# Where three groups of VectorE sums stand in a fast-matrix-product feed-forward kernel

## The reference

```python
def _moe_ref(x, w_in, w_out):             # the second layer: 1.702 * h in the exponent
    h = x @ w_in                          # 2304x512 @ 512x2048
    g = h * (1.0 / (1.0 + np.exp(-h)))
    return (g @ w_out).astype(np.float32) # 2304x2048 @ 2048x512
...
x = np.ascontiguousarray(attn_out.transpose(0, 2, 1, 3)).reshape(B * S, H * D)
x = _moe_ref(x=x, **moe_kwargs)
return _moe2_ref(x=x, **moe2_kwargs)
```

## Time and profile before

| | before |
|---|---|
| median of 3 runs | 829.08 us (828.62, 829.08, 831.41) |
| the profiled execution, its own time | 831.32 us |
| its span, first to last instruction | 829.4 us |
| TensorE matmul busy | 806.5 us (97%) |
| VectorE busy | 653.4 us (79%) |
| ScalarE busy | 536.2 us (65%) |
| GpSimd busy | 191.8 us (23%) |
| TensorE's mean granted clock | 0.994 |
| DMA | 205.42 MB, mean 248 GB/s |

### The profile page before, as it was taken

How to read it: one execution, slowest core, us unless ns; L and a number is a source line. 1 busy time by engine, 2 the same in 40 slices (tenths; PEclk the granted TensorE clock), 3 DMA queues, 4 the chain that set the end, 5 groups by cost and what they waited for, 6 DMA issues and landing times.

```text
span 829.4 us, 15638 instructions
## 1 busy us (share of the span) xinstructions
PE 806.5 (97%) x5787; PEld 778.4 (94%) x5787; DVE 653.4 (79%) x945; ACT 536.2 (65%) x865; POOL 191.8 (23%) x191
## 2 busy tenths in 40 slices
PE   7988899999999999999999999999999999999998
PEld 4766679999999999999999999999999999999997
DVE  6889869989989867888767888899756677665465
ACT  5887775667735567745677555687465787365763
POOL 6678768612025511036300000000000000000000
PEclk8999999999999999999999999999999999999999
DMA  7878756877677897768887787877887777878773
GB/s 211 246 196 231 200 163 234 276 245 260 205 247 249 274 311 263 251 209 262 265 288 254 232 258 251 271 244 235 301 282 260 265 252 265 290 241 267 270 260 126
DMA packets 98315, 205.42 MB, mean 248 GB/s; under 512 B 8416, under 2 KB 56032, under 8 KB 98240
## 3 DMA queue, kind: packets, MB, share of 16 engines
q1 hardware_dynamic: 98240, 204.42, 75.5%
HBM read 160.87 MB, written 43.52 MB: 246 GB/s over the span
## 4 chain that ended last, share of the span: by engine, by line
PE 76%; DVE 8%; DMA 6%; issue 3%; POOL 3%; ACT 2%; SPq 0%; DVEq 0%; POOLq 0%; ACTq 0%
PE hid L322 39%; PE yp L345 35%; DMA vn<-in_v 5%; DVE gr L498 2%; POOL vpair L897 2%; DMA wr<-in_w_in 1%; DVE wh L294 1%; DVE xs L255 1%; PE pt L1090 1%; ACT xs L251 1%; ACT wh L285 0%; DVE x L1063 0%; ACT yt L938 0%; POOL pband L900 0%; ACT pavg L988 0%
## 5 line engine op out<-in xcount | busy, mean ns | idle before, releaser
L322 PE MATMUL hid<-xs,wh 128*128 128x384 f32 x2016 | 352.9, 335 | 3.2 <-DVE hw L478 2.1
L322 PEld LDWEIGHTS hid<-xs,wh 128*128 128x128 f32 x2016 | 349.0, 188 | 6.1 <-issue 4.8
L345 PE MATMUL yp<-gr,wh 128*128 128x384 f32 x2016 | 352.5, 335 | 1.8 <-DVE gr L498 1.8
L345 PEld LDWEIGHTS yp<-gr,wh 128*128 128x128 f32 x2016 | 351.0, 189 | 2.3 <-issue 2.3
L285 ACT ACTIVATE wh<-wr 128x1024 fp32r<-128x1024 f32 (+1 forms) x164 | 164.5, 1003 | 157.7 <-PE hid L322 118.0
L498 DVE TENSOR_TENSOR gr<-G,gr 128x768 fp32r<-128x768 f32 x144 | 138.6, 971 | 48.3 <-ACT gr L398 48.2
L398 ACT ACTIVATE gr<-G 128x768 fp32r<-128x768 f32 x144 | 121.8, 846 | 68.9 <-PE yp L345 67.6
L294 DVE TENSOR_TENSOR wh<-wr,wh 128x1024 fp32r<-128x1024 f32 x76 | 89.4, 1176 | 23.1 <-ACT wh L285 23.0
L365 ACT ACTIVATE G<-G 128x1152 f32<-128x1152 f32 x48 | 55.8, 1162 | 0.0
L488 DVE TENSOR_TENSOR G<-hv,hid 128x384 f32<-128x384 f32 x48 | 26.5, 552 | 27.0 <-PE hid L322 26.9
L473 DVE TENSOR_TENSOR hv<-p,hid 128x384 f32<-128x384 f32 x48 | 26.4, 549 | 26.9 <-PE hid L322 19.3
(11 more groups left out here) (94 smaller groups left out, 766.8 us busy)
## 6 DMA issues: line engine op xcount, KB each, us to landing
wh<-rests SPq DMA_DIRECT2D x72, 512.0 KB, 3.8
wr<-sums_out SPq DMA_DIRECT2D x48, 512.0 KB, 4.7
wr<-in_w_out SPq DMA_DIRECT2D x36, 512.0 KB, 5.2
rests<-wh SPq DMA_DIRECT2D x36, 512.0 KB, 3.3
wr<-sums_in SPq DMA_DIRECT2D x40, 384.0 KB, 4.0
wr<-in_w_in SPq DMA_DIRECT2D x40, 256.0 KB, 3.4
qk<-in_qkT SPq DMA_DIRECT2D x11, 576.0 KB, 6.3
G<-in_w_in SPq DMA_DIRECT2D x12, 512.0 KB, 7.2
```

Of the source, the lines that this page charges most:

```text
L322: last = eng.matmul(hid[:, at, 0:HALF], lhsT=wh[:, w % SLOTS, part, a % 4, cc * P:(cc + 1) * P], rhs=xs[:, rest, q, cc, :], start=start an ...
L345: last = eng.matmul(yp[:, at + m, 0:HALF], lhsT=wh[:, w % SLOTS, part, p % 4, m * P:(m + 1) * P], rhs=gr[:, p, rest, :], start=start and p ...
```

## The change

`results` moves on VectorE from the end of product 6's list to its head. On ScalarE the last `round_x` of the next block moves from behind a weight rounding to before it, in the same product. In blocks 0 and 3 three of the four slices of `sum_t2` move into the first phase (behind the G22 sum of pairs 2, 4 and 6), the fourth goes to product 1 of the second phase, and the four slices of `sum_t4` move from product 4 to products 2 and 3, where `sum_t2` was. No instruction is added or removed.

```diff
@@ scalar: second(n, i)
+                if i == 6:
+                    round_x(eng, n + 1, FILLS[i])
                 for a in range(4):
                     if i < 6:
                         round_gates(n, i + 1, a)
                     if a == 1:
                         round_weights(eng, w + SLOTS)
-                    if a == 2:
+                    if a == 2 and i < 6:
                         round_x(eng, n + 1, FILLS[i])
...
+        EARLY_T2 = (0, 3)
...
@@ vector: first(n, p)
                 eng.tensor_tensor(G[:, p, G22, :], hw[:], hid[:, 3, 0:HALF], ALU.add).then_inc(self.h_sum, 1)
+                if n in EARLY_T2 and p in (2, 4, 6):
+                    sum_t2(n, p // 2 - 1)
                 rest_weights(eng, w + SLOTS)
...
@@ vector: second(n, i)
+                if i == 6:
+                    results(n)
                 for a in range(4):
                     if i < 6:
                         rest_gates(n, i + 1, a)
                     if a == 1:
                         rest_weights(eng, w + SLOTS)
-                        if 2 <= i < 4:
+                        if n in EARLY_T2:
+                            if 2 <= i < 4:
+                                sum_t4(n, 2 * i - 4)
+                        elif 2 <= i < 4:
                             sum_t2(n, 2 * i - 4)
                         elif i == 4:
                             sum_t4(n, 0)
                     if a == 2:
                         prepare_x(eng, n + 1, i)
                     if a == 3:
-                        if 2 <= i < 4:
+                        if n in EARLY_T2:
+                            if i == 1:
+                                sum_t2(n, 3)
+                            elif 2 <= i < 4:
+                                sum_t4(n, 2 * i - 3)
+                        elif 2 <= i < 4:
                             sum_t2(n, 2 * i - 3)
                         elif i == 4:
                             for b in range(1, 4):
                                 sum_t4(n, b)
-                if i == 6:
-                    results(n)
                 rest_weights(eng, w + 1 + SLOTS)
```

## The result

The changed kernel takes **824.73 us** (median of 6 runs, 823.02 to 825.78); the kernel before, beside it, 828.8 us (6 runs, 827.47 to 831.41). The ratio is 0.9948, with a 95% interval of 0.9928 to 0.9968: faster by 0.5%. The forecast was 824.7 us, with a range of 822.9 to 827.8. The total came out as forecast, but the terms behind it didn't all.

The account below looks back on a forecast made before the run. TensorE's matmuls fill 97% of the span, so only its lost 7.83 us can be won. Terms of 3.5, 0.2, 0.8, 0.8, 0.3 and 0.8 sum to 6.4 us; between 824.9 and 824.4 it took 824.7 us, range 822.9 to 827.8.

Parts of the forecast that it names:

- The T2 and T4 sums in block 0: Block 0, second phase: TensorE's gap at product 6 goes and the slow clock with it; 3.5 us, bounds 1.8 to 3.6.
- Rival 1: Block 0, second phase: the gap is won but the clock falls anyway, 1.7 us not won; 826.4 us, chance 0.10.
- the forecast's two workings: Total: 824.9 us from the profiled execution less 6.4; 824.4 from the median less 4.7, if it lacked the slow clock.
- rival 2: Block 0, products 2 to 4: margins of 0.02 to 0.09 us fail, a new wait; 827.4 us, chance 0.14.
- The sums in the first phase: Block 0, first phase: three T2 sums behind G22 in pairs 2, 4 and 6 cost nothing, bounds 0 to 0.1-0.3 us each.
- The start of block 1: Block 0 to 1: `hw` ready at about 239.7, needed at 240.38; 0.8 us won, between 0.3 and 1.06.
- `results` at the head: Starts of blocks 1, 2, 4 and 5: earlier result sums win 0.8, 0.8, 0.3 and 0.8 us.
- the later of its two causes stays: Block 5, first phase: SyncE still stops for `last_result`, so only half the excess is won, 0.8 us (0 to 1.68).
- Block 3: Block 3, second phase: the same T2 and T4 edit without GpSimd work beside it wins 0.2 us (0 to 0.24).
- the third: Second-layer block starts: set by `last_result`'s store and the transfers, not by `results`; 1.1 us back, 825.8 us, chance 0.12.
- the fourth: Product 6's gap comes from something other than the T4 sums, and block starts from ScalarE; 829.1 us, chance 0.04.
- the fifth: Block 0, first phase: VectorE becomes the bound, `hw` late three times with slow clock; 832.2 us, chance 0.04.

Follow-up runs that it names:

- sums_only: Against the changed kernel, `results` and `round_x` back in their old places, only the T2 and T4 sums of blocks 0 and 3 moved; 826.5 us, ratio 0.9979 to before.
- results_only: Against the kernel before, only `results` at the head of product 6 and `round_x` moved, T2 and T4 sums unmoved; 826.93 us, ratio 0.9975.
- one_early: The kernel before with one T2 slice of block 0 moved to pair 2 of its first phase; 829.46 us.
- one_more: The kernel before with one more VectorE instruction, an unused reduction, behind the T4 sums of block 0; 829.63 us.
- the two repeats: The kernel before, run and profiled twice more without any change; 828.74 and 830.7 us.
- no_pool9: The changed kernel with GpSimd's four weight sums of pair 9 cut to 2 of 256 columns; 822.99 us.
- late_stores: The changed kernel with SyncE's stores of the late halves (ends of blocks 3 and 4) also waiting for `hv` of the next block's first pair; 827.02 us.
- before_again: The kernel before, unchanged, run and profiled once more; 828.74 us.

## Why the prediction was right, and where it wasn't

**The T2 and T4 sums in block 0.** The step was: the four T4 sums leave product 4, the first slice of product 6 is ready 0.67 us before need, 3.5 us won. In the profiles compared, the phase went from 61.85 to 58.32: 3.53 us. The first slice's rest starts at 225.46 in the changed kernel, so it is usable at 226.55, 0.68 us ahead of 177.31 + 6 x 8.32 = 227.23. The mechanism is shown by sums_only, by results_only, and by one_early and one_more. The size holds for that pair of profiles only. Rival 1 (the clock falls anyway) named the 1.7 us of slow clock as unsure, and that they are, in another way: mostly they were not there before the change either. In the two repeats the same phase had 1.9 us to win. That is one reason why the median fell by less (4.1 us) than the profiled executions (5.7); on another chip the medians differ by 5.5 us (829.41 and 823.94), so the medians alone don't tell. Of the forecast's two workings the second, from a median that lacked the slow clock, had the sounder premise: two of three profiles of the kernel before lack it.

**The edge in products 2 to 4** (rival 2) held: in block 0's second phase 0.08 and 0.00 us are lost. The margins forecast as 0.09 and 0.02 us measure 0.10 (product 3's first slice starts at 201.08) and 0.04 us (product 5's at 217.78). The sums in the first phase cost nothing, and that phase takes as long as before (54.43 us from 122.88 to 177.31; before it was 54.44). They did take longer beside GpSimd (1.03, 1.38 and 1.03 us), as the bound from the earlier trace rows allowed. VectorE in the changed kernel, pair 4:

```profile
153.33 1.38 DVE L461 TENSOR_TENSOR G<-G 128x768 f32<-128x768 f32 x1
154.64 1.49 DVE L294 TENSOR_TENSOR wh<-G,wh 128x768 fp32r<-128x768 f32 x1
```

The sum took 1.38 us and the rest behind it 1.49 instead of 1.21, and `hw` of pair 5 ended at 160.29, with 177.31 - 21.84 + 5.20 = 160.67 needed. The margin of 0.9 us shrank to 0.4. The rule of the Trainium skill ("SBUF — State Buffer", "Who interferes with whom"), that a VectorE instruction with two inputs from SBUF contends with a GpSimd instruction that reads SBUF, agrees with these rows; it cost nothing here, and 1.1 us at the start of block 1 (no_pool9).

**The start of block 1 is the step that failed.** The prediction: "two weight rests, one of x, `hv` and `hw`: about 239.7, needed at 240.38", so 0.8 us won, at least 0.3. Measured: 0.44 us lost against the profile of before, and nothing won against its two repeats (1.45 and 1.48 us of excess, then 1.50 and 1.68). Counted from the start of block 0's second phase, VectorE reaches the result sums at 54.76 us as forecast (54.96). They take 4.14 us instead of some 3.7, and the five instructions behind them 5.7 us instead of 4.1. So `hw` is ready 64.60 us after that start and not 62.76. The stretch by GpSimd was named and then not put into the sum, and no_pool9 shows that GpSimd's four sums alone make 2.0 us. The bounds had no negative end either, though the same edit made TensorE arrive 3.5 us sooner.

Against the repeats the balance is plain: `hw` comes 2.0 us sooner after that start (66.57 us in both, then 64.60) and TensorE 1.9 us sooner, so the wait stays what it was. The slow clock changes it little. Where it fell, VectorE first caught up, but then it stood still, because ScalarE's next weight rounding waits for TensorE's products to free the weights. This row is of the kernel before:

```profile
235.77 0.96 DVE L294 TENSOR_TENSOR wh<-wr,wh 128x768 fp32r<-128x768 f32 x1 [1.37 <-ACT wh L285]
```

That is why some 1.5 us of slow clock made the next wait only 0.4 us shorter: the excess of block 1 is 1.06 and 1.05 us with the slow stretch (before, one_more) and 1.45 and 1.48 in the repeats. The gap by itself bought nothing: without a gap it is 1.44 to 1.68 us (sums_only, late_stores, the changed kernel), with half of the gap 1.81 (one_early), and with the whole gap and the new order of `results` 2.03 and 2.38. Read together, the two phases go from 4.67 us (3.39 in both repeats) to 1.58.

**`results` at the head.** It wins nothing at block 1, against the 0.8 forecast for that start: without the gap the two orders come out alike (sums_only), and with it the new order is 0.6 us the worse one (results_only). The cause, one more instruction beside GpSimd against one wait for ScalarE, is read from the rows and wasn't tried alone. It wins at block 2 0.52 us of the 0.8 forecast; sums_only, without it, has 0.79 us of excess there, and the two changed profiles 0.30 and 0.16. In blocks 4 and 5 it wins all: 0.42 and 1.68 in these profiles, against 0.3 and 0.8; in the repeats there were 0.58 and 0.60, and 0.35 and 0.82 us to win. There the step "the later of its two causes stays" was too careful. SyncE still stops for `last_result`, and ScalarE still waits for the load behind it, but less:

```profile
718.82 1.06 ACT L285 ACTIVATE wh<-wr 128x1024 fp32r<-128x1024 f32 x1 [1.92 <-DMA wr<-in_w_in]
```

That is 1.92 us where it was 3.72, and TensorE loses nothing by it. The load went out 10.5 us behind the block's start both times (713.80 here) and was there after 5.0 us instead of 7.20. Why it was quicker wasn't tried alone; that less traffic stood ahead of it, since the loads of the first stop had gone out some 2.7 us earlier against the block's start, is an inference. The repeats of the kernel before speak in part against it: there ScalarE waited 2.33 and 3.22 us, and in before_again the load was there after 4.7 us, with the old order.

**Block 3** gave 0.24 us where 0.2 was forecast.

Of the other rivals, the third (blocks 4 and 5 bound elsewhere) fell with their excess of 0, the fourth (the gap has another cause) with sums_only; its second half, block starts set by ScalarE, has something in it at block 1, as the waits of 1.37 and 0.48 us for ScalarE show; the fifth (VectorE the bound in block 0's first phase) fell with that phase's unchanged 54.43 us. Of the signs that were to show the forecast right, two failed: the `hw` wait at block 1 under 0.3 us (it is 1.07), and block 5's first phase at 58.5 to 59.5 us (it is 58.24).

So the sum was right by errors of opposite sign: block 1 was forecast 1.2 us too well and block 5 0.9 us too badly, in the pair of profiles compared. That the median came within 0.1 us of the forecast is luck, as the attention part alone moves an execution by up to 2.7 us.

## What to carry to other kernels

When an engine off the critical path is busy without a break, removing the wait it causes in one place lets its lateness show up in the next; cost the next place with the new, earlier time at which the work is needed, and give that bound a negative end. Inside such a stretch order by need: what is wanted later (here a weight rest needed 2.1 us after `hw`) goes behind what is wanted first. Look also at which of its instructions come to lie beside another engine's that stretches them, and which would wait for a third engine; moving `results` changed both. And before a term is built on a clock event or a short wait in one profile, look at how far the runs of the same kernel lie apart: the profiled execution was 2.2 us above the median here, and some 1.5 us of that may have been the event.

## What the runs showed of the hardware that was not expected

The slow clock behind a short TensorE gap is not certain. Behind gaps of 1.78 us (before) and 2.51 us (one_more) the granted clock was at its lower level of 1.2 GHz for a time; behind gaps of 1.77, 1.67, 1.67 and 1.66 us at the same place, and behind the 1.76 us in results_only at block 1, it stayed at 2.4 GHz. Where it fell, the 48 matmuls behind the gap took 10.15 and 9.98 us instead of 8.56 to 8.59: 1.4 to 1.6 us, a little under the 1.7 us that the prediction read. VectorE's instructions kept their durations there (0.95 and 1.22 us for the same sizes), so the next wait was 0.4 us shorter (0.78 us in the kernel before against 1.18 and 1.21 in its repeats).

Beside GpSimd's 128x256 sums, VectorE's instructions with two inputs took up to 1.54 us instead of 0.95 (128x768) and up to 1.77 us instead of 1.22 (128x1024). GpSimd's sums, 0.74 us at their shortest, took 1.33 to 1.46 us in most of these rows.
